# Last block: quarter-row gathers and VectorE block transposes in place of whole rows and TensorE transposes, with w_in laid out by whole rows

## The reference

```python
# mixture: x is (4, 576, 512); e is the token's expert, p[e] its softmax weight
h = np.maximum(x[b, s] @ w1[e], 0.0)
out[b, s] = p[e] * (h @ w2[e])
# last block: x is the mixture's output, D = 512, D_ff = 1024, K = 3
h = np.maximum(x @ w_in, 0.0)
conv_out = sum(conv_w[k][None, None, :] * hp[:, k:k + S, :] for k in range(K))   # hp: h with one zero token each side
gate = 1.0 / (1.0 + np.exp(-conv_out))
return (h * gate @ w_out).astype(np.float32)
```

## Time and profile before

| | us |
|---|---|
| median of 3 runs | 746.98 (746.82, 746.98, 748.25) |
| span of the profiled execution, first to last instruction | 746.1 |
| the runs above that span | 0.7 to 2.2 |
| PE busy | 735.4 (99%) |
| DVE busy | 432.8 (58%) |
| POOL busy | 329.1 (44%) |
| mean granted TensorE clock | 0.997 |

### The profile page before, as it was taken

One profiled execution on the slowest core, in us unless ns is written; L12 is line 12 of the kernel. 1 busy time (PEld: TensorE's weight loads), 2 busy tenths in 40 slices (PEclk: granted clock), 3 DMA queues, 4 the chain that ended last, 5 costly groups with the idle time before them and its releaser, 6 DMA issues.

```text
span 746.1 us, 15123 instructions
## 1 busy us (share of the span) xinstructions
PE 735.4 (99%) x4971; PEld 626.7 (84%) x4971; DVE 432.8 (58%) x1042; ACT 322.1 (43%) x635; POOL 329.1 (44%) x442
## 2 busy tenths in 40 slices
PE   8999999999989999999999999999999999999998
PEld 6788887887887888888888888888899889889986
DVE  5777878878776544444444545454399455636510
ACT  5777878878430112212121311100397345535620
POOL 7759788887325469444444854400521100000000
PEclk9999999999999999999999999999999999999999
DMA  7888879984064666333334543200421110000011
GB/s 161 206 211 224 230 204 217 239 223 124 17 200 142 232 193 249 144 127 142 127 141 127 171 160 119 89 29 29 139 62 33 43 36 15 29 29 14 29 43 56
DMA packets 99848, 93.39 MB, mean 125 GB/s; under 512 B 62124, under 2 KB 71620, under 8 KB 99780
## 3 DMA queue, kind: packets, MB, share of 16 engines
q1 hardware_dynamic: 79252, 46.51, 22.9%
q10 hardware_dynamic: 17056, 34.69, 13.6%
q0 software_dynamic: 3472, 11.28, 5.3%
HBM read 76.13 MB, written 16.33 MB: 124 GB/s over the span
## 4 chain that ended last, share of the span: by engine, by line
PE 70%; DVE 1%; DMA 0%; issue 0%; ACT 0%; POOLq 0%; DVEq 0%; ACTq 0%
PE row_bank L1306 19%; PE wide_bank L1289 18%; PE wide_bank L1551 14%; PE row_bank L1589 13%; PE wide_bank L1327 3%; PE bank L1255 1%; PE bank L1520 1%; DMA x_slots<-x_rows,token_of 0%; PE bank L1540 0%; PE wide_bank L28 0%; PE row_bank L1540 0%; PE bank L1017 0%; DVE y_sb L1411 0%; DVE xs_tr L1376 0%; DVE xs_tr L1374 0%
## 5 line engine op out<-in xcount | busy, mean ns | idle before, releaser
L912 POOL TENSOR_TENSOR ring<-raw_w,ring 128x2048 fp32r<-128x2048 f32 x28 | 128.6, 4614 | 87.7 <-ACT ring L902 87.7
L1289 PE MATMUL wide_bank<-ring,xs_tr 128*128 x600 | 143.3, 394 | 0.7 <-DVE xs_tr L1368 0.4
L1306 PE MATMUL row_bank<-ring,h_tr 128*128 x600 | 143.5, 394 | 0.0
L902 ACT ACTIVATE ring<-raw_w 128x2048 fp32r<-128x2048 f32 x30 | 55.8, 1908 | 200.3 <-DMA raw_w<-in_moe_w_dram 169.6
L1306 PEld LDWEIGHTS row_bank<-ring,h_tr 128*128 128x128 f32 x600 | 110.8, 188 | 22.7
L1289 PEld LDWEIGHTS wide_bank<-ring,xs_tr 128*128 128x128 f32 x600 | 110.7, 188 | 22.9 <-issue 1.1
L1551 PE MATMUL wide_bank<-x_tr,ring 128*128 128x288 f32 x768 | 107.7, 297 | 0.0
L1551 PEld LDWEIGHTS wide_bank<-x_tr,ring 128*128 128x128 f32 x768 | 103.2, 188 | 0.9
L1589 PE MATMUL row_bank<-ring,g_tr 128*128 128x512 f32 x432 | 100.1, 389 | 0.0
L1589 PEld LDWEIGHTS row_bank<-ring,g_tr 128*128 128x128 f32 x432 | 80.5, 188 | 16.1
L692 ACT ACTIVATE prob<-score,row_min 128x128 f32<-128x128 f32 (+2 forms) x144 | 83.4, 580 | 17.9 <-DVE row_min L555 14.6
(11 more groups left out here) (236 smaller groups left out, 1009.5 us busy)
## 6 DMA issues: line engine op xcount, KB each, us to landing
raw_w<-in_moe_w_dram ACTq DMA_DIRECT2D x12, 2048.0 KB, 8.8
ncum_row<-cum_rows SPq DMA_DIRECT2D x15, 512.0 KB, 5.6
y_sorted<-y_sb SPq DMA_DIRECT2D x26, 256.0 KB
raw_w<-in_moe_w_dram SPq DMA_DIRECT2D x12, 512.0 KB, 3.9
ncum_tail<-cum_rows SPq DMA_DIRECT2D x32, 144.0 KB, 4.4
out_dram<-out_sb ACTq DMA_DIRECT2D x18, 256.0 KB, 2.0
v_nat<-in_v_dram SPq DMA_DIRECT2D x32, 128.0 KB, 3.0
q_nat<-in_q_dram SPq DMA_DIRECT2D x30, 128.0 KB, 4.0
```

Source lines behind the costliest of these rows:

```text
L902: nc.scalar.activation(high, whole, ACT.Copy).then_inc(high_ready, 1)
L912: nc.gpsimd.tensor_tensor(low, whole, high.bitcast(F32), ALU.subtract).then_inc(low_ready, 1)
L1289: last = nc.tensor.matmul(h_bank[:, half, :], xs_tr[:, a, kb, :], ring[:, bass.ds(n, 1), b, at:at + FH].rearrange("p a c -> p (a c)"), sta ...
L1306: last = nc.tensor.matmul(y_bank[:, :], h_tr[:, a, kb, :], ring[:, bass.ds(n, 1), 2 + b, kb * D:(kb + 1) * D].rearrange("p a c -> p (a c)" ...
```

## The change

1. Each token's row in `y_sorted` is seen as four quarters of 512 B. For batches 1 to 3 `gather_quarters` fetches a tile by four indirect DMAs (two for a tail) of 128 offsets each: partition 32g + r of DMA i takes quarter g of token 32i + r. The offsets are the row number times 4 plus g.
2. So each partition needs offsets and weights of other tokens than before. DVE copies the places into `of_token` beside the weights; SP writes this table to a DRAM array `by_row` by four DMAs that store single 4-byte elements (1,280 each), and reads it back by four DMAs of 32 rows after the first two slots' stores. DVE fills a column with g by four small memsets and computes `row_i` in one instruction near the end of the experts.
3. `scale` becomes a multiply of two tensors (128x512, with the weight broadcast over each quarter row), 128x256 for a tail.
4. PE's `turn` is gone. DVE transposes each tile in blocks of 32x32 by one instruction that reads every fourth element of `y_tok` and writes the PSUM bank that PE wrote before. It stands behind `scale`, two jobs ahead of where PE had it.
5. As every fourth element goes to one block, the contraction is over features 4p + kb. So `w_in` is loaded with 4 whole rows on each partition, and the transposes and the last slot's matmuls of batch 0, which stay on PE, take every fourth column of `y_tok` and `y_sb` as their stationary operand.

```diff
+        sp.wait_ge(table_ready, 2)
+        for i in range(QUARTERS):
+            sp.dma_start(by_row[:, :, i], of_token[i * Q:(i + 1) * Q, :, :].rearrange("p n t -> p (n t)"),
+                         allow_slow_non_contiguous=True).then_inc(table_stored, 16)
...
+        def gather_quarters(t):
+            pool.wait_ge(x2_turned, t - TB + 1)
+            for i in range(quarters_of(t)):
+                pool.indirect_dma_start(out=y_tok[t % TB][:, i * P:(i + 1) * P], out_offset=None, in_=y_quarters,
+                                        in_offset=bass.IndirectOffsetOnAxis(ap=row_i[:, t, i:i + 1], axis=0))\
+                    .then_inc(gathered[t % TB], 16)
...
         pool.wait_ge(y_stored, 16 * SLOTS)
+        pool.wait_ge(rows_found, 1)
         for t in range(TB, 2 * TB):
-            gather(t)
+            gather_quarters(t)
         for n in range(len(h_pad)):
             nc.gpsimd.memset(h_pad[n][:, 0:K // 2], 0.0)
             last = nc.gpsimd.memset(h_pad[n][:, K // 2 + S:K - 1 + S], 0.0)
...
+        def every_fourth(rows, kb):
+            return rows.rearrange("p (c k) -> p k c", k=KD)[:, kb, :]
...
         for j in range(2, JOBS):
             b, f = j // KF, j % KF
-            for t in due(j):
-                turn(t)
             above(pe, hp_ready, j - 1)
...
-            V.tensor_scalar(y_tok[t % TB][rows, :], y_tok[t % TB][rows, :], weight[rows, t:t + 1], None, ALU.mult)\
-                .then_inc(x2_ready, 1)
+            V.tensor_tensor(rows, rows, of_row[:, 1, t, 0:n].unsqueeze(2).to_broadcast([P, n, P]), ALU.mult).then_inc(x2_ready, 1)
+
+        def turn(t):
+            n = quarters_of(t)
+            dve.wait_ge(x2_ready, t + 1)
+            above(dve, x2_low, t - TB - 1)
+            V.transpose(bank[t % 2][:, :].rearrange("p (k i r) -> p k i r", k=KD, r=Q)[:, :, 0:n, :],
+                        y_tok[t % TB][:, 0:n * P].rearrange("p (i c k) -> p k i c", k=KD, i=n)).then_inc(x2_turned, 1)
...
             for t in due(j + 2) if j + 2 < JOBS else []:
                 scale(t)
+                turn(t)
             dve.wait_ge(conv_begun, j + 1)
```

More of the change, by code:

```diff
@@ L1157, in vector_weights @@
         then(V.tensor_tensor(weight[:, :], weight[:, :], mass[:, :], ALU.mult))
+        for g in range(QUARTERS):
+            last = V.memset(quarter[g * Q:(g + 1) * Q, :], float(g))
+        last.then_inc(table_ready, 1)
         dve.wait_ge(conv_turned, 1)
@@ L1203, in sync_experts @@
         sp.dma_start(y_sorted[LAST:LAST + P, :], y_sb[:, :]).then_inc(last_zeroed, 16)
-        with sp.Fori(0, SLOTS - 1) as s:
-            sp.wait_ge(y_ready, s + 1)
-            sp.dma_start(y_sorted[bass.ds(s * P, P), :], y_sb[:, :]).then_inc(y_stored, 16)
+        sp.wait_ge(table_ready, 2)
+        for i in range(QUARTERS):
+            sp.dma_start(by_row[:, :, i], of_token[i * Q:(i + 1) * Q, :, :].rearrange("p n t -> p (n t)"),
+                         allow_slow_non_contiguous=True).then_inc(table_stored, 16)
+        for begin, end in ((0, 2), (2, SLOTS - 1)):
+            if begin:
+                sp.wait_ge(table_stored, 16 * QUARTERS)
+                for g in range(QUARTERS):
+                    sp.dma_start(of_row[g * Q:(g + 1) * Q, :, :, :].rearrange("p n t i -> p (n t) i"), by_row[:, :, :])\
+                        .then_inc(table_loaded, 16)
+            with sp.Fori(begin, end) as s:
+                sp.wait_ge(y_ready, s + 1)
+                sp.dma_start(y_sorted[bass.ds(s * P, P), :], y_sb[:, :]).then_inc(y_stored, 16)
         for t in range(TB):
@@ L1427, in vector_experts @@
         relu(SLOTS - 1, (0,))
+        dve.wait_ge(table_loaded, 16 * QUARTERS)
+        V.tensor_scalar(row_i[:, :, :], of_row[:, 0, :, :], float(QUARTERS), quarter[:, 0:1], ALU.mult, ALU.add).then_inc(rows_found, 1)
         V.tensor_scalar(last_row[:, :], place_i[:, 0:TB], -1.0, float(LAST), ALU.mult, ALU.add).then_inc(last_placed, 1)
@@ L1457, in mixture, with quarters_of, landed @@
              (3, TB, (row_bank[0][:, :], bank[0][:, :], bank[1][:, :], row_bank[1][:, :])))
+    y_quarters = y_sorted.rearrange("n (g c) -> (n g) c", g=QUARTERS)
+    def quarters_of(t):
+        return rows_of(t) // Q
+    def landed(t):
+        return 16 + 16 * sum(quarters_of(n) for n in range(t % TB + TB, t + 1, TB))
     pad_ready, in_done, hp_ready, conv_done = sem("pad_ready"), sem("in_done"), sem("hp_ready"), sem("conv_done")
@@ L1512, in pool_block @@
                 if t + TB < T:
-                    gather(t + TB)
+                    gather_quarters(t + TB)
     def tensor_block(pe):
[L1516 to L1522, removed]
+        def every_fourth(rows, kb):
+            return rows.rearrange("p (c k) -> p k c", k=KD)[:, kb, :]
         def first_turn(t, part, blocks=range(KD)):
@@ L1760, in program @@
     y_sorted = dram("y_sorted", (slots * P, D))
+    by_row = dram("by_row", (32, 2 * B * -(-S // P), P // 32))
     with ExitStack() as keep:
@@ L1770, in program @@
         att, mix = mixture(nc, always, keep, region, identity, attend, x_rows, y_sorted,
-                           w_gate, w_local, w1, w2, w_in, conv_w, w_out, out)
+                           w_gate, w_local, w1, w2, w_in, conv_w, w_out, out, by_row)
         keep.callback(region.close)
```

39 lines of the change are left out of this document (24 added, 15 removed).

## The result

The changed kernel takes 790.08 us (median of 5 runs, 789.56 to 790.94) against 746.98 for the one before: ratio 1.0577, interval 1.0565 to 1.0589. The forecast was 763.7 with a range of 757 to 775; the time lies 15 us above the range. The profiled execution took 789.73 us, its span is 788.0.

The account below looks back on a forecast made before the run. PE was taken as the bound (busy 735.4 of 746.1 us). Span 746.1 + 20.3 (last block's delay) - 3.7 (transposes off PE) + 0.1 (routing) = 762.8; the median stands 0.9 above: 763.7, range 757 to 775.

Parts of the forecast that it names:

- I stay by hidden: Experts' stage: the table's stores land by 247, before the slots need them, and cost nothing.
- rival C: Experts' stage: the table's stores hold up the slots, most likely by 3 to 12 us, 767 to 776; chance 12%.
- The other row I had: Table's stores priced by a row of 256 4-byte elements in 6.6 us: 68 us, landed near 304, +48.
- The clock (D): Last block: after 12 us idle, PE's jobs may run at half clock; four would cost 3 us, 766.6; within forecast's 76%.
- POOL's 18 gathers: Last block: 1.255 us each ahead of the border zeroing, so it ends at 556.5, 17 us later; PE idles some 12.
- rival "by bytes" (A): Last block: gather issue time goes by bytes, 0.43 us each, so PE's 6.8 us are gained: 740.2; chance 8%.
- DVE: Last block: scale adds 0.7 us and transposes 5.8, stretching DVE's work from 32.6 to 39.1 us before the first output group.
- B: Last block: POOL is in time but DVE is not, +0.6 us, 747.6, no change; chance 4%.
- Sum of the last block: First output group 20.3 us later, less 3.7 us for later tiles' transposes taken off PE.
- PE's strided stationary loads: Batch 0: at most 4 us if all doubled, hidden in PE's gap of 12 us while POOL gathers.
- Routing: Ahead of the slot table PE waits for: one more cast of 128x20, 0.1 us, bounded by 0 and 0.18.

Follow-up runs that it names:

- e1_runs: Changed kernel with the table stored in 128 runs of 160 bytes instead of 5,120 elements of 4 bytes, and read back in such runs: 779.34 us.
- e6_stores: Kernel before plus only the table's four element-by-element stores to DRAM (5,120 elements of 4 bytes), never read: 774.01 us.
- e7_two: Kernel before plus only two of the table's four DMAs of 1,280 elements of 4 bytes, never read: 765.45 us.
- x1_burst: Kernel before with borders zeroed first and 13 extra unused gathers in an unbroken row behind batch 1's five: 762.88 us.
- x3_paced: Kernel before with borders zeroed first and 13 extra unused gathers behind batch 1's five, with POOL waiting for landings between them: 747.56 us.
- x4_short: Kernel before with borders zeroed first and four extra unused gathers, unbroken, behind batch 1's five: 746.87 us.

## Why the prediction was wrong, point by point

- **What failed: "I stay by hidden", rival C's term.** Forecast: table landed by 247, cost nothing, and 12% for a stall of 3 to 12 us. Its fourth store landed at 261, and it cost 26 us. e1_runs takes the 26 us away (landing back at 533.79) and e6_stores brings them into the kernel before (774.01), so this is shown, from both sides. Two things were wrong in the step. I priced the table by the time of its own packets, 34 ns each, the mean of a queue whose packets average 46.51 MB / 79,252, or 590 bytes. Their own time is even less, 17 ns in e6_stores. But the packets of the gathers beside them took 1.04 us in place of 0.17, and that the sum left out: from 233.7 to the first late landing near 257 the engines spent 23 us x 16 / 5,120 = 72 ns for each element, the delayed neighbours included. And I asked only whether the table itself lands in time, by one wait (slot 0's store); the e7_two run shows that the gathers and weight loads beside it are slowed too and have less slack, with half the elements still costing some 18 us. The other row I had, 256 elements in 6.6 us, gave 68 us and +48; the truth lay between the two, and between ends so far apart 12% for the dearer side was too little. The Trainium skill, DMA: Bandwidth & Descriptors, Specifications, says that transfers below 512 bytes don't reach line rate. The 160-byte runs of e1_runs are below it too and cost nothing ahead of the last block. The same bytes went in 128 pieces in place of 5,120; whether the number of pieces or the size of each decides, no run separates.
- **The clock (D)** was forecast for the last block and is there: granted 0.50 from 584 to 586, 0.78 to 588 and 1.00 after that, and the three jobs behind the gap took 11.21 us where 3 x 3.19 = 9.6, hidden as DVE was behind. It cost more, 4.8 us, behind the two gaps of the experts, where I had no gap.
- **POOL's 18 gathers**: 1.25 us each as forecast, the rival "by bytes" (A) is refuted. ACT's tap 22.55 us behind the landing, forecast (557.4 - 0.78) - 533.7 = 22.9. Right.
- **DVE**: transposes 1.117 and 0.651 us (1.11, 0.63), scaling 0.684 and 0.415 (0.67, 0.33). Right; B falls.
- **Sum of the last block**: +15.8 us, forecast 20.3 - 3.7 = 16.6. Right in size and, in this kernel's trace, step by step. It owes something to luck: with the same order of all engines, e1_runs has 36 us of idle stretches of ACT without a releaser and a last block some 15 us longer. The forecast has no term for these, and why the changed kernel was spared is open.
- **PE's strided stationary loads**: L1565 took 197 to 216 ns (means by shape) where 138 to 141 is the time in order, L1574 some 320 where it was 189. From the landing to ACT's first h_pad it is 8.05 us against 7.16: 0.9 us, hidden in the gap as forecast.
- **Routing**: PE's row behind the slot table began 0.42 us later (forecast 0.1). Small.

## What to carry to other kernels

Count the pieces of a DMA and their size, not its bytes alone, and where a burst of small ones stands beside other transfers, look at every stream that passes through the DMA engines in that stretch and at the slack of each, not only at the queue it is issued on. When two rows bound a price at 0 and +48 us, the run that measures it is cheaper than an argument for one end. Before a gain is booked for removing a wait that a profile names, ask what its absence starts; here other stretches took its place. Before a pattern is blamed for a loss, look for it where nothing was lost: the changed kernel's own trace has the long rows and no stall. Breaking up long rows of POOL's gathers is a cheap thing to try, and no more than that is shown.

## What the runs showed of the hardware

- While 5,120 stores of 4 bytes were under way, the 16 DMA engines had a share of 0.83 to 1.30 for some 23 us and moved 24 to 83 GB/s (before: 0.54 to 0.88, at 157 to 314), and a gather's packet beside them (e6_stores) took 1.04 us in place of 0.17.
- In five runs ACT stood for 6 to 16 us at a time, the bank it took up next full well before (in x1_burst full near 540.9, taken up at 546.58), and in e1_runs PE issued one matmul in two microseconds, all beside unbroken rows of 18 or more indirect gathers of POOL. Thirteen extra gathers cost 15.4 us in a row (x1_burst), and no more than the noise with waits between (x3_paced, 0.6 us) or when there were four (x4_short). The changed kernel has rows of 36 and 18 without it, and the runs with it and those without it are of different chips, so a long row is not enough, and that it is needed is not shown. Runtime: NRT & Kernel Launch of the Trainium skill, section Instruction fetch mechanics, has each engine's sequencer fetch its instructions by a DMA queue of its own and calls the cost of passing from one block to the next "mostly hidden". No packet of instructions is recorded where these stretches end, so the traces give no sign that a late one caused them.
- A transpose on DVE with every fourth element read takes 1.117 us for 128x512; PE's weight load from every fourth column takes 203 to 209 ns against 139 to 141 for the full tiles (L1565, L1531).
